# A third bank for the transposes of P, and the turns of q and k spread over the units of an attention pair

## What is computed

```python
scores = scale * np.matmul(q, k.transpose(0, 1, 3, 2)) + bias
scores = np.where(keep, scores, -1000000000.0)    # keep: the last 96 positions, and the first 8
a = np.exp(scores - np.max(scores, axis=-1, keepdims=True))
a = a / (np.sum(a, axis=-1, keepdims=True) + 1e-09)
x = np.matmul(a, v)                               # (1536, 512) after joining the heads
h = x @ w_in
g = h * np.tanh(softplus(h))
x = g @ w_out
for e in range(4):
    out += p[:, e:e + 1] * (np.maximum(x @ w1[e], 0.0) @ w2[e])
```

## Time and profile before

| | us |
|---|---|
| median of 3 runs | 897.05 (896.2 to 897.34) |
| profiled execution | 896.58 |
| its span on the core | 894.6 |
| attention, to the last output on DVE | 144.7 |

### The profile page before, as it was taken

The page is one execution under the profiler, slowest core; times in us unless marked ns, Lnnn a source line. Parts: engine busy times, 40 slices in busy tenths (PEclk is TensorE's granted clock), DMA queues, the critical chain, the costliest instruction groups (busy, mean ns, idle before and its releaser), DMA issues.

```text
span 894.6 us, 12640 instructions
## 1 busy us (share of the span) xinstructions
PE 866.6 (97%) x4918; PEld 438.7 (49%) x4918; DVE 491.7 (55%) x1016; ACT 309.2 (35%) x580; POOL 260.9 (29%) x222
## 2 busy tenths in 40 slices
PE   7878999999999999999999999999999999999998
PEld 6756776444444444444444444444444444444443
DVE  7878887999999999864432125222144321212121
ACT  5878875554554756541121010201010111101020
POOL 1646995222222222210049100086000392000000
PEclk9999999999999999999999999999999999999999
DMA  9961240000000000202000500002200000000001
GB/s 219 314 200 37 49 177 2 1 0 1 1 7 4 0 1 1 97 19 77 9 1 0 188 1 1 6 0 93 95 1 7 0 0 0 0 36 12 35 12 50
DMA packets 52005, 39.20 MB, mean 44 GB/s; under 512 B 40816, under 2 KB 41712, under 8 KB 51440
## 3 DMA queue, kind: packets, MB, share of 16 engines
q1 hardware_dynamic: 49888, 34.31, 12.7%
q10 hardware_dynamic: 2064, 4.19, 1.3%
HBM read 35.35 MB, written 3.15 MB: 43 GB/s over the span
## 4 chain that ended last, share of the span: by engine, by line
PE 87%; DVE 5%; ACT 5%; issue 2%; POOL 0%; DVEq 0%
PE bank L623 68%; PE bank L696 14%; ACT tmp L867 2%; PE bank L552 2%; ACT tmp L909 1%; PE bank L594 1%; PE bank L613 1%; DVE tmp L1145 1%; ACT scaled L883 1%; DVE wpieces L1094 1%; PE bank L571 1%; DVE xT L1254 1%; PE bank L507 1%; DVE tmp L1273 0%; ACT hid L860 0%
## 5 line engine op out<-in xcount | busy, mean ns | idle before, releaser
L978 ACT ACTIVATE hid<-bank 128x512 f16<-128x512 f32 x96 | 57.3, 597 | 422.2 <-PE bank L623 422.2
L623 PE MATMUL bank<-xT,wA 128*128 128x512 f16 (+1 forms) x864 | 194.6, 379 | 0.0
L1383 DVE SCALAR_TENSOR_TENSOR hid<-bank,hid 128x512 f16<-128x512 f32 x96 | 66.4, 692 | 181.7 <-ACT hid L978 181.7
L623 PEld LDWEIGHTS bank<-xT,wA 128*128 128x128 f16 x864 | 84.5, 98 | 100.6
L696 PE MATMUL bank<-hid,wB 128*128 128x512 f16 x576 | 132.1, 379 | 0.6 <-DVE xT L1254 0.6
L623 PE MATMUL bank<-xT,wB 128*128 x576 | 125.3, 379 | 0.0
L623 PE MATMUL bank<-wB,hid 128*128 128x512 f16 x576 | 125.3, 379 | 0.0
L623 PE MATMUL bank<-wA,hid 128*128 128x512 f16 x576 | 125.3, 379 | 0.0
L790 POOL TENSOR_SCALAR stage<-stage,sc 128x1024 f32<-128x1024 f32 x32 | 36.0, 1125 | 267.9 <-DVEq L1376 250.4
L833 POOL TENSOR_TENSOR tmp<-tmp 128x512 f32<-128x512 f32 x48 | 61.5, 1280 | 179.3 <-DVE tmp L1406 179.3
L1463 DVE SCALAR_TENSOR_TENSOR acc<-bank,pg,acc 128x512 f32<-128x512 f32 x36 | 27.0, 751 | 131.7 <-PE bank L623 131.7
(11 more groups left out here) (115 smaller groups left out, 930.5 us busy)
## 6 DMA issues: line engine op xcount, KB each, us to landing
stage<-in_moe_w SPq DMA_DIRECT2D x8, 2048.0 KB, 9.9
stage<-in_moe_w_in SPq DMA_DIRECT2D x1, 4096.0 KB, 14.4
wB<-in_moe_w_out ACTq DMA_DIRECT2D x1, 4096.0 KB, 16.6
hid<-in_q SPq DMA_DIRECT2D x16, 192.0 KB, 3.5
hid<-in_k SPq DMA_DIRECT2D x16, 192.0 KB, 3.5
xT<-in_v SPq DMA_DIRECT2D x8, 384.0 KB, 5.1
out_y<-acc SPq DMA_DIRECT2D x12, 256.0 KB, 2.0
rows<-max SPq DMA_DIRECT2D x4, 128.0 KB, 4.2
```

Of the source, the lines that this page charges most:

```text
L623: last = pe.matmul(dst, lhs(c, a), rhs(c, b), start=(c == 0 and n == 0), stop=(c == chunks - 1 and n == 2))
L978: act.activation(hv[:, f, 0, :], psum(f % 4), ACT.Relu).then_inc(f_hi, 1)
L1383: dve.scalar_tensor_tensor(hv[:, f, 1, :], psum(f % 4), 0.0, hv[:, f, 0, :], ALU.max, ALU.subtract).then_inc(f_ready, 1)
```

## The change

It has three parts.

In pairs 1 to 6, P is turned into three banks (4, 5 and 3 by u % 3) instead of two; in pairs 4 to 6 only in units 0 to 5, since bank 3 is needed for the x turn in unit 8. `turn` waits for the two readers of the last unit that used the bank.

The four fills of pairs 2 to 7 go. Instead each unit of pairs 1 to 6 turns one tile of the next pair into the last 128 columns of the bank in which its P is turned, ahead of P. Units with even u turn q, those with odd u turn k. ACT copies the tile ahead of its copy of P; every fourth unit (`at % 4 == 1`) DVE copies it instead, behind its remainder. The scores of a pair wait for the tiles that they need. `tr_psum`, on which SP's loads wait, now rises behind units 2, 5, 8 and 11.

The pieces of the two maxima come every 2.5 units on the average, by turns on ACT and DVE (before: every 2 for w_in, every 3 for w_out). The maximum of w_in is spread with the scores of unit 46 (was: with the turn of unit 40), into the free columns of a score bank, and its scale is made in unit 45 (was 41); for w_out these are unit 66 (was 65) and 65 (was 66).

```diff
-        W_ACT = [[start + gap * c for c in range(PIECES // 2)] for start, gap in ((2 * UNITS - 2, 4), (4 * UNITS - 8, 6))]
-        W_DVE = [[at + gap for at in units] for units, gap in zip(W_ACT, (2, 3))]
+        W_ACT = [[start + 5 * c for c in range(PIECES // 2)] for start in (2 * UNITS - 2, 4 * UNITS - 6)]
+        W_DVE = [[at + 2 for at in units] for units in W_ACT]
...
-        W_SHARE = ({n: at + 3 for n, at in W_MAX[0].items()}, {0: UNITS + 9})
+        W_SHARE = ({n: at + 6 for n, at in W_MAX[0].items()}, {0: UNITS + 9})
...
+        def p_bank(at):
+
+            m, u = divmod(at, UNITS)
+            two = m in (0, PAIRS - 1) or (m >= PAIRS - 4 and u >= UNITS // 2)
+            return 4 + u % 2 if two else (4, 5, 3)[u % 3]
...
+        def tile_at(at):
+
+            m, u = divmod(at, UNITS)
+            return (u % 2, u // 2, (m + 1) % 2) if 1 <= m < PAIRS - 1 else None
...
+        def tile_on_dve(at):
+
+            return at % 4 == 1
+
+        def tile_psum(at):
+
+            return psum(p_bank(at), P, 3 * P)
...
@@ score_parts
+                elif banded and 2 * i + slot >= 2:
+                    if u % 2 == 0:
+                        wait_tiles((2 * i + slot - 1) * UNITS + u + 1)
...
@@ scores_of_two
+                for n, unit in W_SHARE[0].items():
+                    if (2 * i + slot) * UNITS + u == unit:
+                        share_max(n, psum(u % 3, P, 3 * P))
...
+            def wait_split(at):
+
+                pe.wait_ge(pT_act, at + 1)
+                pe.wait_ge(pT_dve, at + 1)
+                wait_tiles(at)
...
@@ turn
-                if banded and at >= 2:
-                    pe.wait_ge(pT_act, at - 1)
-                    pe.wait_ge(pT_dve, at - 1)
                 if banded:
-                    for n, unit in W_SHARE[0].items():
-                        if at == unit:
-                            share_max(n, psum(4 + u % 2, P, 3 * P))
+                    used = p_bank_before(at, p_bank(at))
+                    if used is not None:
+                        wait_split(used)
...
+                    tile = tile_at(at)
+                    if tile:
+                        j, t, to = tile
+                        if u == 0:
+                            pe.wait_ge(qk_loaded[to], 64 * ((2 * i + slot + 1) // 2 + 1))
+                        moved = pe.transpose(tile_psum(at), nat[to][j][:, t * P:(t + 1) * P], ident[:])
+                        if u % 3 == 2:
+                            moved.then_inc(tr_psum, 1)
...
@@ pair on PE
-                    if after(i, slot) and u in FILL_AT:
+                    if after(i, slot) and u in FILL_AT and (not banded or before(i, slot) is None):
                         fill(*after(i, slot), FILL_AT.index(u), banded)
...
@@ x turn on PE
-                        pe.wait_ge(tr_out, FILLS * min(2 * i + slot + 2, PAIRS))
+                        if banded:
+                            wait_split(p_bank_before((2 * i + slot) * UNITS + u + 1, 3))
...
@@ ACT
+            def copy_tile(at):
+
+                if not tile_at(at) or tile_on_dve(at):
+                    return
+                j, t, to = tile_at(at)
+                if j == 0:
+                    m = at // UNITS + 1
+                    last = act.activation(qT_sb[to][:, t * P:(t + 1) * P], tile_psum(at), ACT.Copy,
+                                          scale=q_scale[:, m:m + 1])
+                else:
+                    last = act.copy(kT_sb[to][:, t * P:(t + 1) * P], tile_psum(at))
+                last.then_inc(tile_act, 1)
...
                     act.wait_ge(pT_psum, PB * i + UNITS * slot + u + 1)
-                    src, pt = p_out(u, banded)
+                    if banded:
+                        copy_tile((2 * i + slot) * UNITS + u)
+                    src, pt = p_out(i, slot, u, banded)
...
@@ DVE
-                    if banded and at == W_SHARE[0][n] + 1:
+                    if banded and at == W_SHARE[0][n] - 1:
                         matrix_scale(n)
...
+                    at = (2 * i + slot) * UNITS + u
+                    if banded and tile_at(at) and tile_on_dve(at):
+                        _, t, to = tile_at(at)
+                        dve.tensor_copy(kT_sb[to][:, t * P:(t + 1) * P], tile_psum(at)).then_inc(tile_dve, 1)
```

More of the change, by code:

```diff
@@ L255, in program @@
         tr_out = sem("tr_out")
+        tile_act, tile_dve = sem("tile_act"), sem("tile_dve")
         s_psum = sem("s_psum")
@@ L375, in reach, with p_bank_before, p_out @@
             return other and (*other, (u + ahead) % UNITS)
-        def p_out(u, banded):
+        def p_bank(at):
+            m, u = divmod(at, UNITS)
+            two = m in (0, PAIRS - 1) or (m >= PAIRS - 4 and u >= UNITS // 2)
+            return 4 + u % 2 if two else (4, 5, 3)[u % 3]
+        def p_bank_before(at, this):
+            return max((n for n in range(at) if p_bank(n) == this), default=None)
+        def p_out(i, slot, u, banded):
             if not banded:
@@ L381, in p_out, with tiles_out @@
             n = len(band[u // 2]) * P
-            return psum(4 + u % 2, n), pT_b[u % 3][:, :, 0:n]
+            return psum(p_bank((2 * i + slot) * UNITS + u), n), pT_b[u % 3][:, :, 0:n]
+        def tile_at(at):
[5 more added lines that the diff above has]
+            return psum(p_bank(at), P, 3 * P)
+        def tiles_out(at):
+            tiles = [n for n in range(UNITS, at + 1) if tile_at(n)]
+            on_dve = sum(tile_on_dve(n) for n in tiles)
+            return len(tiles) - on_dve, on_dve
         def fill_cols(k):
@@ L540, in score_parts, with wait_tiles @@
                         for key, n, at in runs]
+            def wait_tiles(at):
+                by_act, by_dve = tiles_out(at)
+                if by_act:
+                    pe.wait_ge(tile_act, by_act)
+                if by_dve:
+                    pe.wait_ge(tile_dve, by_dve)
             def scores(i, slot, u, banded):
@@ L583, in turn @@
                 src = s_b[u % 3] if banded else s_g
-                dst, _ = p_out(u, banded)
+                dst, _ = p_out(i, slot, u, banded)
                 at = UNITS * (2 * i + slot) + u
-                if banded and at >= 2:
-                    pe.wait_ge(pT_act, at - 1)
-                    pe.wait_ge(pT_dve, at - 1)
                 if banded:
-                    for n, unit in W_SHARE[0].items():
-                        if at == unit:
-                            share_max(n, psum(4 + u % 2, P, 3 * P))
+                    used = p_bank_before(at, p_bank(at))
+                    if used is not None:
+                        wait_split(used)
+                    elif p_bank(at) == 3:
+                        pe.wait_ge(tr_out, FILLS * 2)
+                        pe.wait_ge(v_scale, 2)
+                    turned = sum(n < at for n in X0_BANDED)
+                    if p_bank(at) == 3 and turned:
+                        pe.wait_ge(x_ready, turned)
+                    tile = tile_at(at)
[6 more added lines that the diff above has]
+                            moved.then_inc(tr_psum, 1)
                 for b in range(len((band if banded else full)[u // 2])):
@@ L912, in pair @@
                         expo(*ahead, banded)
-                    if following and u - 1 in FILL_AT:
+                    if following and u - 1 in FILL_AT and (not banded or before(i, slot) is None):
                         copy_out(*following, FILL_AT.index(u - 1))
@@ L1143, in biased @@
                     dve.wait_ge(s_psum, UNITS * m + u + 1)
+                    for n, unit in W_SHARE[0].items():
+                        if UNITS * m + u == unit:
+                            matrix_max(n, psum(u % 3, P, 3 * P))
                     dve.sem_inc(carrier, 1)
```

13 lines of the change are left out of this document (4 added, 9 removed).

## The result

| | before | changed |
|---|---|---|
| median of 6 runs | 897.06 us (896.2 to 898.9) | 903.75 us (903.56 to 905.79) |
| profiled execution | 896.58 us | 903.79 us |
| its span on the core | 894.6 us | 901.9 us |
| attention, to the last output on DVE | 144.7 us | 152.1 us |

The changed kernel takes 1.0077 of the time of the one before, 95% interval 1.0064 to 1.0091: 6.7 us slower. I had forecast 896.4 and a range up to 900.5, so the time is outside it. All of it is lost by the end of the attention: the last output step starts at 151.58 us instead of 144.16, 7.4 later, and the spans differ by 7.3.

What follows compares the result with a forecast made beforehand. PE was taken to bound pairs 1 and 6, the ACT-DVE exchange pair 2, with pairs 3 to 5 mixed. Tiles -0.2 and x turn -0.4 gave -0.6, other terms 0: median 896.4 us, forecast range 895 to 898.5, overall 893.0 to 900.5.

Steps and rivals of the forecast that it cites:

- What bounds it: Attention pairs: PE sets the pace in pairs 1 and 6, ACT and DVE in pair 2, pairs 3 to 5 mixed.
- rival (b): Small copies stand in the line between ACT and DVE in pairs 2 to 5: +4.9, 901.9 us; chance 0.28.
- Pieces of the maxima: Sixteen pieces before and after, two moving between pairs: 0, with anything from -1.4 to +1.4 us possible.
- Tiles instead of fills: Pairs 1 to 6: old fills taken off the chain, new work charged by each engine's old chain share: -0.2 us.
- the x turn's wait: Pair 5's x turn no longer waits for a copy of k, 0.8 us of PE; half counted, -0.4 us.
- my -0.2: Sum over pairs 1 to 6 of replacing fills by tiles, in us, before the x turn's -0.4.
- The estimate of about +1: Five more ACT instructions per pair at 172 cycles cost 0.7 us; sum about +1 us instead of -0.6.
- the third bank: Turn of P: the old wait goes but the exponential still holds the turn; 0, ends 0 and -1.6 us.
- the passed waits: Some 36 more PE wait instructions per pair for tiles, none holding: 0, upper end 2 us over six pairs.
- The later scale: First scale 6.0 us later, POOL's splits ending at 151.6, 0.6 late: hidden, with 0.7 us left.
- First product right behind the last split: Sign of the forecast: POOL's last split at 151 to 152 and its first product right behind.
- Rival (a): PE's waits were the cause and the decoupling pays: -4.7, 892.3 us, or 894.3 with half of them; chance 0.28.

Runs made afterwards that it cites:

- e1: Kernel before with only the pieces of the maxima at the new units and the scales moved along: 900.62 us, 1.0058 of the kernel before.
- e10: Kernel before with two of sixteen pieces moved, from units 58 and 61 to 57 and 59, scales in their old units: 900.29 us, 1.0043.
- e2: Changed kernel with the pieces and scales back at their old units: 899.18 us, 1.0028 of the kernel before.
- e5: Changed kernel without its 72 tile copies: 899.90 us, 1.0038 of the kernel before.
- e6: Kernel before without ACT's 24 fill copies for pairs 2 to 7: 893.76 us, 0.9970 of the kernel before.
- e3: Changed kernel with two banks for P in every unit: 902.82 us, 1.0075 of the kernel before.
- e14: Changed kernel without the waits for tiles that another wait implies: 904.06 us, 1.0081 of the kernel before.
- e12: Changed kernel with PE's wait for the exponential moved behind the tile's transpose: 903.90 us, 1.0073 of the kernel before.
- e4: Changed kernel with ACT copying the tile one unit later, behind the exponential: 902.10 us, 1.0064 of the kernel before.
- e17: Changed kernel with pieces cut to 128 of 1024 columns and without its 72 tile copies: 891.80 us, 0.9951 of the kernel before.
- e18: Kernel before with pieces cut to 128 of 1024 columns and without ACT's 24 fill copies: 886.62 us, 0.9891 of the kernel before.
- e11: Changed kernel with the last two pieces of w_out put back to units 58 and 61: 901.39 us, 1.0049 of the kernel before.

## Why the prediction was wrong

**What bounds it.** The reading of the pairs was right as a description of before: pair 2, where I forecast 17 to 18 us, took 17.48 with five pieces instead of six. But ACT's lines in its chain are 48% where I had named over 60, pair 1 took 13.71, where I had written 13.2, and pair 6 took 14.80 with PE on 44.5% of its chain, which I had named as a sign of rival (b).

**Pieces of the maxima: the step that failed most.** I took a price per piece and pair (1.3 and 0.6 us), saw as many pieces before as after, and put 0 with ends of 1.4 either way. Measured, the new units cost 5 us (e1), and two pieces moved by one and two units cost 3.8 (e10). The price of a piece isn't a mean over its pair. It depends on what stands beside it in its unit: in e10 the x turn's copies and the output step; that the short units at the turn of a pair, where little work covers it, have a part in it is my reading and not shown. (The 0.6 was also too low by its own rows: pair 1 has one piece, L883 in the earlier trace rows, so pair 4 has three more, not four, which gives 0.7.) The row that could have said so was the timeline of ACT and DVE at 93 to 99 us, and I had not laid the units of the new pieces beside it.

**Tiles instead of fills: right in the lengths of the copies, wrong in its sum.** The copies took 0.358 us for q and 0.257 for k on ACT, and 0.281 on DVE, as these groups by shape say:

```profile
L932 ACT ACTIVATE hid<-bank,q_scale 128x128 f32<-128x128 f32 x35 | 12.5, 358 | 5.5 <-PE bank L653 5.3
L1353 DVE COPY hid<-bank 128x128 f32<-128x128 f32 x18 | 5.1, 281 | 0.0
L935 ACT COPY hid<-bank 128x128 f32<-128x128 f32 x18 | 4.6, 257 | 0.0
```

0.35 and 0.25 were forecast. But I charged them with the share that their engine had on the chain before the change, as if the chain stayed. In pairs 1 and 6 I charged ACT's copies with 19 and 4%; afterwards PE holds only 45% of the chain there. The tile part as a whole, forecast at -0.6 with the x turn's wait, cost 2.5 (e2). Of this the copies are 0.8, by ratios that don't exclude my -0.2 (e5, e6), and with small pieces they cost no more than the old ones (1.9 and 2.1). So rival (b) had the direction of the tile part and its signs in pair 6, but not the cause: its price of 4.9 was for the copies. "VectorE: DVE Perf Modes" of the Trainium skill, section on the TRN2 errata, which I had weighed against the rows, asks for tiles of at least 512 elements; it says so of operations that read SBUF, and these copies read a bank. The estimate of about +1 that I drew from its 172 cycles was also too high: five times 0.143 us instead of 0.3 us per pair, with ACT's shares in the six pairs (218% together), adds 0.9 to -0.6 and gives +0.3. No run shows that the number of copies is what costs.

**What stays open.** Of the tile part, the third bank (e3), the passed waits (e14) and the tile's place ahead of the exponential's wait (e12) are each worth nothing that can be told, the place ahead of P on ACT about 1 us (e4) and the copies 0.8, both within the intervals of none. So with full pieces about 0.5 us of the 2.5 has no candidate that was tested, and no single cause found is clear of noise. The trace of e2, of its slowest execution (900.14 us), has 2.1 us of its loss in one place: from the last output step of pair 2 to that of pair 3 it takes 18.70 us instead of 16.59. Its half clock lies there too, and PE is busy for all of the 4 us from 76. With small pieces it is clearer: 2.7 us of the attention are lost without any copy at all (e17 and e18), and the piece units, the banks and the place of the transposes differ there. A candidate is that PE's turns of tiles now stand between an exponential and its P in 12 units of a pair, where the fills stood in four. No run took the transposes alone away, so this is argued and not shown.

**The rest.** Third bank 0 and new waits 0: nothing that can be told was measured for either (e3, e14). The wait of the x turn for a copy of k is gone, as said, but what I counted for it (-0.4) doesn't show: pair 5 took 2.4 us longer. The later scale is hidden: right with full pieces; with small ones 2.4 us were lost behind the attention (e17 and e18). The scale came 7.2 us later instead of 6.0, since everything before it had slipped as well, and POOL's last split and first product of the changed kernel are

```profile
150.60 2.13 POOL L858 TENSOR_TENSOR wB<-scaled,wB 128x1024 f16<-128x1024 f32 x1
158.10 1.27 POOL L895 TENSOR_TENSOR tmp<-tmp 128x512 f32<-128x512 f32 x1 [5.37 <-DVE tmp L1486]
```

POOL waits the same 5.37 us for DVE ahead of its first product as in the earlier trace rows: it isn't the bound. "First product right behind the last split" was wrong, since the attention ended 7 us later. Rival (a) is excluded: taking PE's waits away bought nothing, new ones took their place. "Perfetto Trace Analysis" of the Trainium skill, section Optimizing Scalar/DVE Operations, says that breaking up instructions may let work complete sooner where ACT and DVE aren't saturated but cause bubbles on other engines. ACT was 77% busy in pair 2 and the copies were broken up; the tile part cost 2.5 us (e2), and no run here shows a gain from it.

**The chances.** The range was too narrow because I gave the move of the pieces ends of 1.4 us, where 5 were in it, and held it apart from rival (b): 901.9 plus a part of those 5 would have reached the result.

## What to carry to other kernels

Where two engines hand each other the work, price a moved instruction by the timeline of its new unit: what stands ahead of it, who waits for what stands behind it, and whether the other engine has its own extra work close behind. A share of the chain prices work only as long as the chain stays where it is: in pair 1, where PE was busy for 13.2 of 13.4 us and ACT for 12.1, PE went from 73% of the chain to 45.5 and the pair became 0.3 us longer, not 0.24 shorter. Waits taken away from an engine that wasn't on the chain were replaced by others.

## What the runs showed of the hardware

Two things I had not expected. DVE steps with all operands outside the banks are held up by POOL's splits until the operation of the split that runs ends: 2.50 and 2.60 us instead of 0.69 for two operands (e17), 1.64 instead of 0.43 for one (e18), while a step with one operand in a bank took its 0.69 beside the same split. And in the changed kernel the granted clock of TensorE fell to 0.50 for some 3.5 us after PE had waited for 1.07, 1.06 and 0.99 us in close order; PE was then busy for 3.75 of 4 us. In e11 and e2 executions with such a stretch took at most 0.5 us more than those without or with less of it; in e10 the lower mean clocks went with up to 3.8 us more.
